# Two pairs of steps at a time in the attention loop of a fused attention, expert and gated kernel

## The chip, the cores and the metric

The kernel runs on one core of one Trainium2 chip. The metric is the device time of one execution in microseconds (us); lower is better. TensorE (PE) multiplies and transposes, VectorE (DVE) and ScalarE (ACT) do elementwise work, GpSimd (POOL) helps, and SyncE (SP) starts most transfers. Each engine takes its own instructions in the order in which they were written and waits for the others by semaphores.

## What is computed

The reference is attention with a window, then a layer in which each token goes to one of eight experts, then a gated layer. The part that the change touches is the attention and the choice of experts that hangs on it:

```python
scores = scale * np.matmul(q, k.transpose(0, 1, 3, 2))       # (4, 8, 768, 768), head_dim 64
keep = is_global | is_local                                  # 8 global keys, 96 local ones
scores = np.where(keep, scores + bias, -1000000000.0)        # bias: -slope of the head * distance
a = np.exp(scores - np.max(scores, axis=-1, keepdims=True))
a = a / (np.sum(a, axis=-1, keepdims=True) + 1e-09)
x = np.matmul(a, v)                                          # then 3072 tokens x 512
...
skip_score = x @ w_skip                                      # tokens with a positive one go on
e_idx = np.argmax(x @ w_gate, axis=1)
y = gate_w * (np.maximum(x @ w1[e], 0.0) @ w2[e])            # expert e of each token
...
return (gate * val @ w_out)                                  # gate, val: products of x with two weights
```

## The kernel before

**Steps and pairs.** The queries are cut into blocks of 128 rows. A step is one block of two heads. A batch has 24 steps (4 pairs of heads, 6 blocks each), and the four batches have 96. Two steps in a row are a pair, 48 pairs in all. Each block sees 256 keys (its own 128, 96 before it, 32 of the start); the first block of every pair of heads, step 0 of each six, sees only its own 128, so its products and elementwise work are half as wide. "Narrow step" means such a one below. Of three pairs in a row two hold a narrow step.

**What a pair goes through.** `scores(m)` (line 1785) makes the products of the two steps of pair m, eight matmuls that use 64 rows of the array each, two at a time (L1797). DVE's `lowest_of` (L911) adds the bias to a step's scores and takes the minimum of each row, into `score` and `lowest`. ACT's `exp_of` (L1510) makes `prob` and the sum of each row. `prob_transposes` (L1807) transposes a step's `prob` on PE, four transposes of 128x128. ACT's `pt_evac` (L1530) copies them to `probT`. `values(m)` (L1823) multiplies them with the values of the two heads, sixteen matmuls with 64 columns of the array each, two at a time, into `o_bank`. DVE's `take_heads_x` (L1117) copies that to `heads_x`. `turn(m)` (L1837) turns it to token rows and makes the expert scores in the same four matmuls, into `turned`. DVE's `take_rows` (L1011, L1131) reads `turned`, multiplies with the inverse sums (`guard_sums` L1107, `invert_sums` L1111) and stores to `head_logit` and `xs`.

**What sets the order.** It is written out by hand. PE's loop takes, for pair m: the scores of pair m+1, the transposes of pair m-1, the turn of pair m-2, the values of pair m-1. DVE takes two `lowest_of`, the sums of pair m-1, the rows of pair m-2, the copy of pair m-1. ACT takes two `pt_evac` of pair m-1 and two `exp_of` of pair m.

**What is shared.** `score`, `prob`, `probT` and `lowest` have a place for each of two steps; `lowest_of` of step n waits for the exp of step n-2. The four score places in PSUM (`sp_bank`) hold two pairs. `pt_bank` has two places: transposes of step n wait for `pt_evac` of step n-2 (`ptev_done`). `turned` is there once: `turn(m)` waits for the rows of pair m-1 (`oev_done`). The sums have two places, by pair: the exps of pair m wait for `guard_sums` of pair m-2 (`norm_chain`).

**Beside it**, per batch from the second on: `add_logits`, `choose` in three parts (seven small DVE instructions), `gate_exp` on ACT, `ranks` on PE (seven small matmuls, L1844 and L1846) with `take_ranks` and `gates` on DVE, all for the batch before. In the first batch `first_bias` and `window_bias` (L888) make the biases of the next pair of heads, after step 3 of each six.

## Time and profile before

| | |
|---|---|
| median of 3 runs | 966.11 us (966.04 to 967.0) |
| the profiled execution | 966.12 us, its span 964.5 us |
| around the span | 1.62 us |
| attention, from the first values to the last turn | 14.4 to 180.3 us of the span |
| PE, DVE, ACT busy over the whole span | 99%, 68%, 53% |
| PE, DVE, ACT busy from 20 to 170 us | 100%, 78%, 85% |
| granted PE clock | 1.00 throughout |

The expert layer and the gated layer follow the attention; they are not touched. PE's matmuls are pipelined and their ends are modelled, so a PE that is busy all the time by the table can still lose time between two kinds of matmul; that is read from the starts of single matmuls. In the rows below PE's time for a group of matmuls is therefore taken from start to start.

### The profile page before, as it was taken

The page shows a single profiled execution, that of the slowest core. Times are in us where ns is not written, and L with a number is a line of the kernel's source. Part 1 is how long each engine was busy: PE and PEld are TensorE (multiplying, and loading weights), DVE is VectorE, ACT ScalarE, POOL GpSimd, SP SyncE. Part 2 cuts the span into 40 slices and gives each one's busy share as a digit, 9 for nine tenths or more (in the row PEclk, how much of TensorE's full clock was granted, in tenths as well). Part 3 has the DMA queues.
Part 4 walks back from the last instruction along what each step waited for, and adds up shares of the span by engine and source line. Part 5 has one row for each costly group of instructions (what it writes and reads, how often), then busy time and mean ns, then how long its engine had stood idle before and what let it go on. Part 6 is the DMA issues. An engine that isn't in the chain of part 4 may idle for free.

```text
span 964.5 us, 16852 instructions
## 1 busy us (share of the span) xinstructions
PE 953.8 (99%) x5638; PEld 799.4 (83%) x5639; DVE 653.8 (68%) x1522; ACT 511.8 (53%) x1086; POOL 206.0 (21%) x229
## 2 busy tenths in 40 slices
PE   8999999999999999999999999999999999999998
PEld 6777777789999999788888888888888888888887
DVE  6887877675666266587677766676777846766653
ACT  5888888444444144364455554454555634545443
POOL 2405142722211111212323000323220013232100
PEclk9999999999999999999999999999999999999999
DMA  7677675689777265442211244512123432120242
GB/s 259 248 303 263 250 265 202 234 299 338 286 255 250 66 240 196 141 142 69 66 47 55 85 130 132 164 45 66 48 66 94 133 121 66 44 66 12 86 138 93
DMA packets 59660, 146.14 MB, mean 152 GB/s; under 512 B 6336, under 2 KB 12480, under 8 KB 59584
## 3 DMA queue, kind: packets, MB, share of 16 engines
q1 hardware_dynamic: 52624, 120.92, 37.5%
q0 software_dynamic: 6960, 24.27, 7.3%
q8 instruction: 40, 0.66, 0.3%
q14 instruction: 36, 0.29, 0.1%
HBM read 116.77 MB, written 28.40 MB: 151 GB/s over the span
## 4 chain that ended last, share of the span: by engine, by line
PE 96%; DVE 1%; DMA 1%; ACT 1%; issue 0%; SPq 0%; DVEq 0%; POOLq 0%; ACTq 0%
PE bank L2034 35%; PE bank L1781 14%; PE bank L1783 14%; PE bank L1782 14%; PE bank L1797 5%; PE bank L1807 5%; PE bank L1823 5%; PE bank L1837 2%; PE bank L2024 1%; PE bank L1962 1%; PE bank L1947 1%; DMA raw<-in_qk_dram 0%; DMA xq<-mixed 0%; PE bank L2087 0%; ACT prob L1510 0%
## 5 line engine op out<-in xcount | busy, mean ns | idle before, releaser
L2034 PE MATMUL bank<-xh,ws_h 128*128 128x512 f32 x490 | 190.6, 389 | 0.0
L2034 PE MATMUL bank<-xl,ws_h 128*128 128x512 f32 x490 | 190.6, 389 | 0.0
L2034 PE MATMUL bank<-xh,ws_l 128*128 128x512 f32 x490 | 190.6, 389 | 0.0
L845 POOL TENSOR_TENSOR p<-p,p 128x512 f32<-128x512 f32 x35 | 46.3, 1324 | 387.6 <-DVE p L1411 387.6
L1781 PE MATMUL bank<-woh,hh 128*128 128x512 f32 x288 | 112.9, 392 | 0.0
L1783 PE MATMUL bank<-woh,hl 128*128 128x512 f32 x288 | 112.2, 389 | 0.0
L1782 PE MATMUL bank<-wol,hh 128*128 128x512 f32 x288 | 112.1, 389 | 0.0
L2034 PEld LDWEIGHTS bank<-xh,ws_l 128*128 128x128 f32 x490 | 92.0, 188 | 19.1
L2034 PEld LDWEIGHTS bank<-xh,ws_h 128*128 128x128 f32 x490 | 92.0, 188 | 19.1
L2034 PEld LDWEIGHTS bank<-xl,ws_h 128*128 128x128 f32 x490 | 92.0, 188 | 19.1
L1510 ACT ACTIVATE prob<-score,lowest 128x256 f32<-128x256 f32 (+1 forms) x192 | 91.3, 482 | 6.2 <-DVE lowest L911 6.2
L1781 PE MATMUL bank<-sTh,w1h 128*128 128x256 f32 x288 | 80.7, 280 | 0.1
L1782 PE MATMUL bank<-sTl,w1h 128*128 128x256 f32 x288 | 80.4, 279 | 0.0
L1783 PE MATMUL bank<-sTh,w1l 128*128 128x256 f32 x288 | 80.4, 279 | 0.0
L1385 DVE TENSOR_TENSOR hl<-hid,hh 128x512 fp32r<-128x512 f32 x72 | 49.6, 689 | 44.1 <-ACT hh L1681 44.0
L1681 ACT ACTIVATE hh<-hid 128x512 fp32r<-128x512 f32 x72 | 45.2, 628 | 51.6 <-PE bank L1783 49.0
L1571 ACT ACTIVATE hTh<-bank 128x512 fp32r<-128x512 f32 x36 | 21.4, 595 | 90.4 <-PE bank L1783 89.9
L1530 ACT ACTIVATE probT<-bank 128x512 f32<-128x512 f32 (+1 forms) x96 | 51.0, 560 | 27.0 <-PE bank L1807 26.1
L911 DVE CUSTOM_DVE_ANT_0 score<-bank,bias_win 128x256 f32<-128x256 f32 x160 | 59.9, 421 | 7.9 <-issue 5.1
L1783 PEld LDWEIGHTS bank<-woh,hl 128*128 128x128 f32 x288 | 54.1, 188 | 11.4
L1781 PEld LDWEIGHTS bank<-woh,hh 128*128 128x128 f32 x288 | 54.1, 188 | 11.3 <-issue 0.5
L1782 PEld LDWEIGHTS bank<-wol,hh 128*128 128x128 f32 x288 | 54.1, 188 | 10.9
(266 smaller groups left out, 2005.5 us busy)
## 6 DMA issues: line engine op xcount, KB each, us to landing
wraw<-in_w_dram SPq DMA_DIRECT2D x64, 512.0 KB, 5.9
graw<-in_w_gated_dram SPq DMA_DIRECT2D x36, 512.0 KB, 3.6
woraw<-in_w_out_dram SPq DMA_DIRECT2D x72, 256.0 KB, 2.6
raw<-in_qk_dram SPq DMA_DIRECT2D x48, 336.0 KB, 6.2
vs<-in_own_prev_dram SPq DMA_DIRECT2D x16, 768.0 KB, 5.2
mixed<-xs SPq DMA_DIRECT2D x12, 512.0 KB, 3.2
xq<-mixed SPq DMA_DIRECT2D x12, 512.0 KB, 6.0
out_dram<-ostage SPq DMA_DIRECT2D x22, 256.0 KB, 2.0
```

What stands on the lines that cost most here:

```text
L845: pool.tensor_tensor(p7[:], p7[:], p1[:], ALU.add).then_inc(u3_done, 1)
L911: ins = dve.tensor_tensor_reduce(out=score[s % 2][:, t, lo:hi], in0=sp_bank[s % 4][t][:, lo:hi], in1=bias, scale=-HD ** -0.5, scalar=3e38, ...
L1385: dve.tensor_tensor(hl[u % 3][:], hid[:, c, h * HALF:(h + 1) * HALF], hh[u % 3][:].bitcast(f32), ALU.subtract).then_inc(hl_done, 1)
L1510: ins = act.activation(prob[s % 2][:, t, lo:hi], score[s % 2][:, t, lo:hi], ACT.Exp, bias=lowest[:, s % 2, t:t + 1], scale=-1.0, accum_out ...
L1530: act.activation(probT[n % 2][:, :, lo:2, :], pt_bank[n % 2][:].rearrange("p (t w c) -> p t w c", t=2, w=2)[:, :, lo:2, :], ACT.Copy).then ...
L1781: pe.matmul(dst, a_hi, b_hi, start=start, stop=False)
L1782: pe.matmul(dst, a_hi, b_lo, start=False, stop=False)
L1783: return pe.matmul(dst, a_lo, b_hi, start=False, stop=stop)
L1797: ins = pe.matmul(sp_bank[s % 4][t][:, lo:hi], both[half, i * P:(i + 1) * P], both[half, end - (hi - lo):end], start=True, stop=True)
L1807: ins = pe.transpose(pt_bank[n % 2][:, (2 * t + w) * P:(2 * t + w + 1) * P], prob[n % 2][:, t, w * P:(w + 1) * P], ident[:])
L1823: ins = pe.matmul(o_bank[t * HD:(t + 1) * HD, i * P:(i + 1) * P], vs[pr % 2][:, 1 - w, t, qi, :], probT[i][:, t, w, :], start=(w == 1 or q ...
L2034: ins = pe.matmul(bank, w[:, a + k], x[:, q, k], start=(first and k == 0 and i == 0), stop=(k == 1 and i == 2), skip_group_check=not first)
```

## The change

The loops of all three engines take two pairs (four steps) per turn, called a group below; a batch has 6 groups, and three groups in a row hold two narrow steps. PE takes the scores of two pairs (four steps), the transposes of the first two of the four steps before, the turn of a pair, the transposes of the third step, the turn of the next pair, the transposes of the fourth step, and the values of two pairs. DVE takes one copy of two pairs (128x512), four `lowest_of`, the sums of one pair, the rows of one pair, the sums of the next, the rows of the next. ACT takes four `pt_evac` and then four `exp_of`. `score`, `prob`, `probT` and `lowest` get four places instead of two, `heads_x` is one tensor of four blocks, and the values use the whole of `o_bank`. `pt_bank`, `turned` and the sums keep their places. The parts of `choose` stand behind the first three `lowest_of` of the batch's third group, the ranks in its fourth group. The semaphores' counts follow. After the last group the rest is written out.

```diff
@@ -118,7 +118,7 @@
-        lowest = small("lowest", [P, 2, 2], f32)
+        lowest = small("lowest", [P, 4, 2], f32)
...
+        more_probT = [till_ranks(f"probT{i}", [P, 2, 2, P], f32) for i in (2, 3)]
+        more_prob = [till_ranks("prob2", [P, 2, KW], f32, end=SMALL + 2 * UNIT + 4 * NQ * SLOT)]
...
-        heads_x = [att2(f"heads_x{i}", [P, 2, P], f32) for i in range(2)]
+        both_heads_x = att2("heads_x", [P, 2 * 2 * P], f32)
...
+        GROUPS = PAIRS // 2
+        CHOOSE, RANK, ROWS = 1, 3, 6
...
@@ -902,15 +912,15 @@
                 lo, hi = windows(qi)
                 n = STEPS * b + s
                 dve.wait_ge(s_done, n // 2 * 2 + 2)
-                if n >= 2:
-                    dve.wait_ge(exp_done, n - 1)
+                if n >= 4:
+                    dve.wait_ge(exp_done, n - 3)
                 alone(dve)
                 for t in range(2):
                     h = 2 * pr + t
                     bias = bias_0[:, h, :] if qi == 0 else bias_win[:, h, :]
-                    ins = dve.tensor_tensor_reduce(out=score[s % 2][:, t, lo:hi], in0=sp_bank[s % 4][t][:, lo:hi],
+                    ins = dve.tensor_tensor_reduce(out=score[s % 4][:, t, lo:hi], in0=sp_bank[s % 4][t][:, lo:hi],
                                                    in1=bias, scale=-HD ** -0.5, scalar=3e38, op0=ALU.add, op1=ALU.min,
-                                                   accum_out=lowest[:, s % 2, t:t + 1])
...
+            def take_heads_x(m, pairs):
+                dve.wait_ge(pv_done, m + pairs)
                 if m >= 2:
-                    dve.wait_ge(turned_done, m - 1)
-                dve.tensor_copy(heads_x[m % 2][:].rearrange("p s r -> p (s r)"), o_bank[:, 0:2 * P])\
-                   .then_inc(heads_x_in, 1)
+                    dve.wait_ge(turned_done, m + pairs - 2)
+                at = m % 2 * 2 * P
+                dve.tensor_copy(both_heads_x[:, at:at + 2 * P * pairs], o_bank[:, at:at + 2 * P * pairs])\
+                   .then_inc(heads_x_in, pairs)
...
-            def pair_after(m):
-
-                b, g = m // PAIRS, m % PAIRS
-                if 1 <= m <= NB * PAIRS:
-                    guard_sums(m - 1)
-                if 1 <= m <= NB * PAIRS:
-                    invert_sums(m - 1)
-                if m >= 2:
-                    take_rows(m - 2, (lambda: take_ranks(b)) if b and g == RANK else None)
-                if b and b < NB and g == CHOOSE:
-                    add_logits(b)
-                if b and b < NB and CHOOSE < g <= CHOOSE + 3:
-                    choose(b, g - CHOOSE - 1)
-                if b and g == RANK + 1:
-                    gates(b)
-                if 1 <= m <= NB * PAIRS:
-                    take_heads_x(m - 1)
+            def sums_inverted(m):
+                guard_sums(m)
+                invert_sums(m)
 
             def body(b):
+
                 if b == 1:
                     dve.wait_ge(const_ready, 1)
-                for s in range(STEPS):
-                    pr = s // NQ
-                    if b == 0 and pr and s % NQ < 2:
-                        dve.wait_ge(bias_done, 2 * pr + s % NQ + 1)
-                    if b or s > 1:
-                        lowest_of(b, s)
-                    if b == 0 and s % NQ == NQ - 3 and pr + 1 < NPAIR:
-                        first_bias(pr + 1)
-                        window_bias(pr + 1)
-                    if s % 2:
-                        pair_after(PAIRS * b + s // 2)
+                for g in range(GROUPS):
+                    m = PAIRS * b + 2 * g
+                    if m >= 4:
+                        take_heads_x(m - 4, 2)
+                    for s in range(4 * g, 4 * g + 4):
+                        pr = s // NQ
+                        if b == 0 and pr and s % NQ < 2:
+                            dve.wait_ge(bias_done, 2 * pr + s % NQ + 1)
+                        if b or s > 1:
+                            lowest_of(b, s)
+                        if b == 0 and s % NQ == NQ - 3 and pr + 1 < NPAIR:
+                            first_bias(pr + 1)
+                            window_bias(pr + 1)
+                        if b and g == CHOOSE + 1 and s % 4 < 3:
+                            choose(b, s % 4)
+                    if m >= 2:
+                        sums_inverted(m - 2)
+                    if m >= 4:
+                        take_rows(m - 4, (lambda: take_ranks(b)) if b and g == RANK else None)
+                    if m >= 2:
+                        sums_inverted(m - 1)
+                    if m >= 4:
+                        take_rows(m - 3)
+                    if b and g == CHOOSE:
+                        add_logits(b)
+                    if b and g == RANK:
+                        gates(b)
             batches(dve, body)
-            for m in range(NB * PAIRS, NB * PAIRS + 2):
-                pair_after(m)
+            end = NB * PAIRS
+            take_heads_x(end - 4, 2)
+            sums_inverted(end - 2)
+            take_rows(end - 4)
+            take_heads_x(end - 2, 1)
+            take_rows(end - 3)
+            sums_inverted(end - 1)
+            take_rows(end - 2)
+            take_heads_x(end - 1, 1)
+            take_rows(end - 1)
...
-                    ins = act.activation(prob[s % 2][:, t, lo:hi], score[s % 2][:, t, lo:hi], ACT.Exp,
-                                         bias=lowest[:, s % 2, t:t + 1], scale=-1.0,
+                    ins = act.activation(prob[s % 4][:, t, lo:hi], score[s % 4][:, t, lo:hi], ACT.Exp,
+                                         bias=lowest[:, s % 4, t:t + 1], scale=-1.0,
...
                 act.wait_ge(pt_done, n + 1)
-                if n >= 2:
-                    act.wait_ge(pv_done, n // 2)
+                if n >= 4:
+                    act.wait_ge(pv_done, n // 2 - 1)
                 lo = 1 if n % NQ == 0 else 0
-                act.activation(probT[n % 2][:, :, lo:2, :],
+                act.activation(probT[n % 4][:, :, lo:2, :],
...
             def body(b):
-                for g in range(PAIRS):
-                    m = PAIRS * b + g
-                    for i in range(2):
-                        if m >= 1:
-                            pt_evac(2 * m - 2 + i)
-                    for i in range(2):
-                        if m:
-                            exp_of(b, 2 * g + i)
-                    if b and g == CHOOSE + 2:
-                        gate_exp(b)
+                for g in range(GROUPS):
+                    n = STEPS * b + 4 * g
+                    for i in range(4):
+                        if n:
+                            pt_evac(n - 4 + i)
+                    for i in range(4):
+                        if n + i > 1:
+                            exp_of(b, 4 * g + i)
+                        if b and g == CHOOSE + 1 and i == 1:
+                            gate_exp(b)
             batches(act, body)
-            for i in range(2):
-                pt_evac(STEPS * NB - 2 + i)
+            for i in range(4):
+                pt_evac(STEPS * NB - 4 + i)
...
-                if m >= 1:
+                if m >= 2 and m % 2 == 0 or m == NB * PAIRS - 1:
                     pe.wait_ge(heads_x_in, m)
                 for i in range(2):
+                    at = (m % 2 * 2 + i) * P
                     qi = first + i
                     pe.wait_ge(ptev_done, 2 * m + i + 1)
                     for w in range(0 if qi else 1, 2):
                         for t in range(2):
-                            ins = pe.matmul(o_bank[t * HD:(t + 1) * HD, i * P:(i + 1) * P], vs[pr % 2][:, 1 - w, t, qi, :],
-                                            probT[i][:, t, w, :], start=(w == 1 or qi > 0) and (w == 0 or qi == 0),
+                            ins = pe.matmul(o_bank[t * HD:(t + 1) * HD, at:at + P], vs[pr % 2][:, 1 - w, t, qi, :],
+                                            probT[(2 * m + i) % 4][:, t, w, :], start=(w == 1 or qi > 0) and (w == 0 or qi == 0),
                                             stop=(w == 1))
                 ins.then_inc(pv_done, 1)
...
             def body(b):
-                for g in range(PAIRS):
-                    m = PAIRS * b + g
-                    if m + 1 < NB * PAIRS:
-                        scores(m + 1)
+                for g in range(GROUPS):
+                    m = PAIRS * b + 2 * g
+                    for i in range(2):
+                        if m + i:
+                            scores(m + i)
                     if m == 0:
                         keep_busy(4)
-                    if m >= 1:
-                        prob_transposes(2 * m - 2)
-                        prob_transposes(2 * m - 1)
-                    if m == 2:
+                    if m >= 2:
+                        prob_transposes(2 * m - 4)
+                        prob_transposes(2 * m - 3)
+                    if m == 4:
                         pe.wait_ge(router_loaded, 16)
                         pe.wait_ge(turner_ready, 1)
+                    if m >= 4:
+                        turn(m - 4, (lambda: ranks(b)) if b and g == RANK else None)
                     if m >= 2:
-                        turn(m - 2, (lambda: ranks(b)) if b and g == RANK else None)
-                    if m >= 1:
+                        prob_transposes(2 * m - 2)
+                    if m >= 4:
+                        turn(m - 3)
+                    if m >= 2:
+                        prob_transposes(2 * m - 1)
+                        values(m - 2)
                         values(m - 1)
                     if m == PAIRS:
                         pe.wait_ge(const_ready, 1)
             batches(pe, body)
             last = NB * PAIRS
+            prob_transposes(2 * last - 4)
+            prob_transposes(2 * last - 3)
+            turn(last - 4)
+            values(last - 2)
+            turn(last - 3)
             prob_transposes(2 * last - 2)
             prob_transposes(2 * last - 1)
             turn(last - 2)
```

How the rows stand on the engines, in the middle of the second batch. On PE, before, one pair and a half: L1797 scores, L1807 transposes, L1837 turn, L1823 values.

```order
L1807 MATMUL bank<-ident,prob_135 128x128 x4
L1807 MATMUL bank<-ident,prob_136 128x128 x4
L1837 MATMUL bank<-turner,heads_x_149 128x146 x2
L1823 MATMUL bank<-probT_137,vs_125 64x128 x4
L1823 MATMUL bank<-probT_138,vs_125 64x128 x4
L1797 MATMUL bank<-raw_132 128x256 x4
L1807 MATMUL bank<-ident,prob_135 128x128 x4
L1807 MATMUL bank<-ident,prob_136 128x128 x4
L1837 MATMUL bank<-turner,heads_x_148 128x146 x2
L1823 MATMUL bank<-probT_137,vs_125 64x128 x4
L1823 MATMUL bank<-probT_138,vs_125 64x128 x4
```

On PE, after, one group: L1819 scores (the second pair's), L1829 transposes, L1860 turn, L1846 values.

```order
L1819 MATMUL bank<-raw_135 128x256 x4
L1829 MATMUL bank<-ident,prob_138 128x128 x4
L1829 MATMUL bank<-ident,prob_139 128x128 x4
L1860 MATMUL bank<-turner,heads_x 128x146 x2
L1829 MATMUL bank<-ident,prob_124 128x128 x4
L1860 MATMUL bank<-turner,heads_x 128x146 x2
L1829 MATMUL bank<-ident,prob_162 128x128 x4
L1846 MATMUL bank<-probT_140,vs_128 64x128 x4
L1846 MATMUL bank<-probT_141,vs_128 64x128 x4
L1846 MATMUL bank<-probT_122,vs_128 64x128 x4
L1846 MATMUL bank<-probT_123,vs_128 64x128 x4
L1819 MATMUL bank<-raw_129 128x256 x4
```

Eight changes between kinds of matmul in two pairs become seven, but of those between different shapes of the array (64x128, 128x128, 128x64) six become three; the second turn stands behind the first with one step of transposes between them.

On DVE, before: the end of one `lowest_of`, the sums and rows of a pair, the copy, the next `lowest_of` (L911; each of its reads has a row of its own).

```order
L911 ISA score_134,lowest<-bank,bias_win 128x256 [waits s_done,exp_done]
L911 ISA lowest 128x1
L911 ISA score_134,lowest<-bank,bias_win 128x256
L911 ISA lowest 128x1
L1107 TENSOR_REDUCE rsum<-sums 128x4 [waits exp_done]
L1111 RECIPROCAL rsum<-rsum 128x4 [waits norm_chain]
L1011 TENSOR_TENSOR head_logit<-bank,rsum 128x2x2x9 [waits turned_done,norm_chain]
L1131 TENSOR_TENSOR xs_143<-bank,rsum 128x2x128
L1117 COPY heads_x_148<-bank 128x256 [waits turned_done,pv_done]
L911 ISA score_133,lowest<-bank,bias_147 128x128 [waits exp_done,const_ready,s_done]
```

On DVE, after: the fourth `lowest_of` of a group (L921), then sums, rows, sums, rows.

```order
L921 ISA score_161,lowest<-bank,bias_win 128x256 [waits s_done,exp_done]
L921 ISA lowest 128x1
L921 ISA score_161,lowest<-bank,bias_win 128x256
L921 ISA lowest 128x1
L1117 TENSOR_REDUCE rsum<-sums 128x4 [waits exp_done]
L1121 RECIPROCAL rsum<-rsum 128x4 [waits norm_chain]
L1021 TENSOR_TENSOR head_logit<-bank,rsum 128x2x2x9 [waits turned_done,norm_chain]
L1142 TENSOR_TENSOR xs_146<-bank,rsum 128x2x128
L1117 TENSOR_REDUCE rsum<-sums 128x4 [waits exp_done]
L1121 RECIPROCAL rsum<-rsum 128x4 [waits norm_chain]
L1021 TENSOR_TENSOR head_logit<-bank,rsum 128x2x2x9 [waits turned_done,norm_chain]
L1142 TENSOR_TENSOR xs_146<-bank,rsum 128x2x128
```

The rows of the first pair (L1021, L1142) now stand behind four `lowest_of` instead of two.

On ACT, before, two pairs: L1530 copies of transposes, L1510 exps.

```order
L1530 ACTIVATE probT_137<-bank 128x512
L1530 ACTIVATE probT_138<-bank 128x512
L1510 ACTIVATE prob_135,sums<-score_133,lowest 128x256 x2
L1510 ACTIVATE prob_136,sums<-score_134,lowest 128x256 x2
L1530 ACTIVATE probT_137<-bank 128x512
L1530 ACTIVATE probT_138<-bank 128x512
L1510 ACTIVATE prob_135,sums<-score_133,lowest 128x128 x2
L1510 ACTIVATE prob_136,sums<-score_134,lowest 128x256 x2
```

On ACT, after, one group: L1552 and L1532.

```order
L1552 ACTIVATE probT_140<-bank 128x512
L1552 ACTIVATE probT_141<-bank 128x512
L1552 ACTIVATE probT_122<-bank 128x512
L1552 ACTIVATE probT_123<-bank 128x512
L1532 ACTIVATE prob_138,sums<-score_136,lowest 128x128 x2
L1532 ACTIVATE prob_139,sums<-score_137,lowest 128x256 x2
L1532 ACTIVATE prob_124,sums<-score_156,lowest 128x256 x2
L1532 ACTIVATE prob_162,sums<-score_161,lowest 128x256 x2
```

All four exps of a group now stand behind the copy of the fourth step's transposes.

## Rows read from the trace of the kernel before

**Rows 1.** Busy time by stretch: stretch, then each engine's busy us (instructions), clock.

```profile
20.00:170.00 150.00, 150.00 (x1485) 118.74 (x1485) 117.66 (x600) 126.88 (x434) 47.15 (x59) 1.00 0.70 250
170.00:180.00 10.00, 8.35 (x83) 6.33 (x80) 6.39 (x31) 7.29 (x24) 9.82 (x7) 1.00 0.40 147
```

**Rows 2.** The chain of waits, three pairs: start us, us, what.

```profile
81.71 1.06 PE bank L1797 x8
...
85.32 1.06 PE bank L1797 x8
...
92.01 0.41 PE bank L1797
```

**Rows 3.** Instructions in order of time, PE: start us, us, engine, line, operation, count.

```profile
81.96 0.59 PE L1797 MATMUL bank<-raw 64*128 64x256 f32 x3
...
82.17 0.60 PE L1797 MATMUL bank<-raw 64*128 64x256 f32 x4
...
82.87 0.49 PE L1807 MATMUL bank<-ident,prob 128*128 128x128 f32 x3
...
83.63 0.41 PE L1837 MATMUL bank<-turner,heads_x 128*128 128x146 f32 x2
...
83.76 0.54 PE L1837 MATMUL bank<-turner,heads_x 128*128 128x146 f32 x3
84.22 0.55 PE L1823 MATMUL bank<-probT,vs 128*64 128x128 f32 x6
...
84.49 0.50 PE L1823 MATMUL bank<-probT,vs 128*64 128x128 f32 x6
```

**Rows 4.** Instructions in order of time, DVE, one narrow and one whole pair.

```profile
82.10 0.28 DVE L911 CUSTOM_DVE_ANT_0 score<-bank,bias 128x128 f32<-128x128 f32 x1
...
85.36 0.42 DVE L1117 COPY heads_x<-bank 128x256 f32<-128x256 f32 x1 [0.43 <-PE bank L1823]
85.71 0.41 DVE L911 CUSTOM_DVE_ANT_0 score<-bank,bias_win 128x256 f32<-128x256 f32 x1
...
87.08 0.16 DVE L1107 TENSOR_REDUCE rsum<-sums 128x4 f32<-128x8 f32 x1
87.27 0.18 DVE L1111 RECIPROCAL rsum<-rsum 128x4 f32<-128x4 f32 x1
87.80 0.20 DVE L1011 TENSOR_TENSOR head_logit<-bank,rsum 128x36 f32<-128x36 f32 x1 [0.35 <-PE bank L1837]
87.91 0.41 DVE L1131 TENSOR_TENSOR xs<-bank,rsum 128x256 f32<-128x256 f32 x1
```

**Rows 5.** Instructions in order of time, ACT: copies of transposes, exps.

```profile
83.39 1.08 ACT L1530 ACTIVATE probT<-bank 128x512 f32<-128x512 f32 x2 [0.62 <-PE bank L1807]
...
84.36 0.40 ACT L1510 ACTIVATE prob<-score,lowest 128x128 f32<-128x128 f32 x1
...
87.72 0.50 ACT L1510 ACTIVATE prob<-score,lowest 128x256 f32<-128x256 f32 x1
...
88.70 0.49 ACT L1510 ACTIVATE prob<-score,lowest 128x256 f32<-128x256 f32 x1
...
89.59 0.18 ACT L1510 ACTIVATION_READ_ACCUMULATOR prob<-score,lowest 128x1 f32 x1
```

**Rows 6.** Instructions in order of time, DVE: a minimum that waited for that exp.

```profile
89.95 0.42 DVE L911 CUSTOM_DVE_ANT_0 score<-bank,bias_win 128x256 f32<-128x256 f32 x1 [0.20 <-issue]
```

**Rows 7.** Instructions in order of time, DVE, first batch: biases, then the sums behind them.

```profile
12.83 0.49 DVE L888 SCALAR_TENSOR_TENSOR bias<-dist 128x128 f32<-128x128 f32 x2
...
13.91 0.15 DVE L1107 TENSOR_REDUCE rsum<-sums 128x4 f32<-128x8 f32 x1
```

**Rows 8.** Instructions in order of time, PE: start and end of the attention.

```profile
19.02 1.14 PE L1797 MATMUL bank<-raw 64*128 64x256 f32 x8
...
171.63 0.92 PE L1823 MATMUL bank<-probT,vs 128*64 128x128 f32 x12
...
179.86 0.77 PE L1837 MATMUL bank<-turner,heads_x 128*128 128x146 f32 x4 [0.53 <-DVE heads_x L1117]
```

19 lines of the change are left out of this document (12 added, 7 removed).

## The prediction

> **What bounds the kernel now.** I read four views in this order. First the busy time by stretch: from 20 to 170 us PE is busy for all 150 us, ACT for 126.88 and DVE for 117.66, at a clock of 1.00 [rows 1]. So PE sets the pace of the attention, and the two others have 15% and 22% to spare. Second the chain of waits: it runs through PE's scores, transposes, turn and values in turn, with 3.61 us from the scores of one pair to those of the next (81.71 to 85.32) and 10.30 for three pairs, two of them with a narrow step (81.71 to 92.01) [rows 2]. Two pairs take 6.87 us on average. Third the starts of single matmuls inside one whole pair [rows 3]; a row with xN starts N matmuls, so its first number is the start of the first. Fourth DVE's and ACT's instructions in order of time, for their lengths and for the delay from one engine to the next [rows 4 to 6].
>
> **What a pair costs on PE.** Slots, from start to start [rows 3]: scores 0.21 to 0.22 per two matmuls (81.96 to 82.17), 0.216 taken; transposes 0.109 (82.87 to 83.63 is seven); turn 0.125 (83.63, 83.76); values 0.109 per two matmuls, the same 128 columns. A whole pair is 4 x 0.216 + 8 x 0.109 + 4 x 0.125 + 8 x 0.109 = 3.11 us. The other 0.50 of the 3.61 is lost where the shape of the array changes. From turn to values: the last turn starts at 84.01, the third double matmul of the values at 84.49, and 0.48 less 0.125 and two slots is 0.14. From scores to transposes: 82.39 to 82.87, less 0.216 and two slots with rounding, 0.15. From values to scores the rest, 0.20.
>
> **What the change takes away.** Two pairs have each of these three seams once instead of twice: 0.50 us per group. With 24 groups that is 12.0 us. This holds only if nothing new makes PE wait, and the next part says that something does. The four places for scores, probabilities and transposes remove waits that are short today, the larger buffers cost nothing, and the single copy of 512 columns (two of 0.42 today [rows 4]; between 0.42 and 0.84, I take 0.7) ends before the new scores can be read.
>
> **What the change adds: a wait at the second turn.** `turned` exists once. The second turn of a group waits until DVE has taken the rows of the first, and on DVE these rows stand behind the copy and all four minima of the group. Lengths: a minimum 0.69 per step (85.71 to 87.08 is two); sums 0.37 (87.08 to the end of the reciprocal); rows 0.53 (87.80 to 88.32) [rows 4]. Delay from PE's last start to DVE 0.32 (the last values start at 85.04, the copy at 85.36). I take 0.06 from DVE back to PE; no row isolates it, 0 to 0.1 bounds it.
>
> *The loop through DVE*, from one second turn to the next, all steps whole: turn 0.50, transposes 0.44, seam 0.14, values 16 x 0.109 = 1.74, seam 0.20, four slots of scores up to the last start 0.65, delay 0.32, four minima 2.74, sums 0.37, rows 0.53, back 0.06: 7.69 us. *The loop through ACT*: turn 0.50, last transpose starting 0.33 later, delay to ACT 0.32, copy 0.49 (two take 1.08 less the overlap, 83.39 to 84.36), four exps 3 x 0.98 + 1.07 = 4.01 (87.72, 88.70, end 89.77), to the minimum that waits for the last exp 0.17 (89.95), that minimum 0.69, sums 0.37, rows 0.53, back 0.06: 7.47 us [rows 5, 6]. PE itself would need 6.22 + 0.50 = 6.72. So either loop is longer than PE's work, and today's 7.22 for two whole pairs too.
>
> A narrow step takes 0.22 from its values, 0.21 from its scores where it stands in the group's first pair, 0.27 from its minimum (0.28 against 0.42 [rows 4], twice) and 0.2 from its exp (0.40 against 0.50 [rows 5], twice). Three groups in a row have a narrow step at their start, in their third step, and nowhere. Over three intervals DVE's loop then gives 7.42 (a narrow minimum), 7.47 (narrow values), 6.99 (all three), and ACT's 7.27, 7.27, 7.47. The longer one decides: 7.42 + 7.47 + 7.47 = 22.36 us against 20.60 today. The attention has 22 such intervals between its first and last full group: 164.0 against 151.1, **+12.9 us**.
>
> **What loses its cover.** Today DVE's extra work hides beside PE; in the new order it stands between minima or behind them, in the loop that decides. Biases of the first batch, two sets inside the intervals, 1.08 each (12.83 to 13.91 [rows 7]): +2.2. `choose`, seven small instructions of some 0.18 (the reciprocal [rows 4]), three times: +3.8. Ranks: their seven matmuls (7 x 0.109, about 0.8) lie on PE's path today and beside DVE's loop then; instead `take_ranks` and `gate_exp` enter it, three small instructions, some 0.6: -0.2, three times, -0.6. `add_logits` and `gates` stand behind the second rows, where DVE waits for the values anyway: nothing.
>
> **Start and end.** Today the first two pairs' values are done by 19.0 us [rows 8]. In the new order the exps of steps 2 and 3 no longer stand behind two copies, but the second pair of scores does stand ahead of the first transposes; between -1 and +1, I take -0.5. At the end, today, 7.4 us lie between the end of the last values but two (some 172.5) and the last turn (179.86) [rows 8]. In the new order the last four exps end 2.8 us after the values of the last full group, a copy of transposes starts at 2.7, values at 3.4 to 4.4, two transposes and a turn to 6.4, the last copy of transposes ends at 6.7, values at 7.6, DVE's copy at 8.3: +1.0. The work behind the attention waits for this last turn and moves with it.
>
> Sum: 12.9 + 2.2 + 3.8 - 0.6 - 0.5 + 1.0 = +18.8 us. The profiled execution took 966.12 us (its span 964.5 and 1.62 around it, which I leave as it is), and the median is 966.11: 984.9.
>
> **Rivals.** *PE's seams decide, 954.1.* If the second turn didn't have to wait, the gain of 12.0 would stand. For it: the seams are in the rows, and DVE and ACT are idle 22% and 15% of the stretch. Against it: the idle time is there on average, but the loops above have their delays in series. It decides once both loops are under 6.7 us, one whole microsecond shorter than worked out. The Trainium skill, page TensorEngine Tiling, section Key Properties, says that changing the tiling mode drains TensorE; the seams of this trace, 0.14 to 0.20, agree with it, and by that rule alone the change is a gain.
>
> *Both loops are shorter, 966 to 976.* If DVE's loop is 0.5 shorter than I have it (shorter handoffs), ACT's still holds: 22 intervals at 7.34 are 161.4, +10.3, and with the other terms 982. Only if ACT's is 0.3 shorter as well do they fall to 7.04 and the time to about 976. No row supports it.
>
> *The clock falls, about 1010.* PE would stand still for about 1 us in each group. Should the granted clock go to 1.2 GHz for a sixth of the stage, four groups' PE work of 6.7 us doubles: +27. Against it: from 170 to 180 us PE was busy 8.35 of 10 us and the clock stayed at 1.00 [rows 1]. On that the Trainium skill, page TensorE: Matmul & The Clock Gate, section HAM oscillation, has a rule that idle gaps between matmul bursts lower the clock; here no row shows it.
>
> *The change does nothing, 966.* Only if loop and seams cancel: intervals of 6.9 and all extra work hidden. I see no reason.
>
> **Chances.** Forecast 0.80; seams decide 0.08; in between, faster or slower, 0.07; the clock or a longer loop 0.05. The unknown terms (handoffs 0.05 x 22, start 1, choose 1, copy 0) make the likeliest case 979 to 992; I give 976 to 994. Faster by over 0.2% 0.09, within 0.2% 0.03 (0.2%, some 2 us, is about what a measurement can tell), slower 0.88.
>
> **What would show it.** Right: the transposes and values of a group are separated from the turn by a wait of PE for DVE's `xs` at the second turn, some 1 us in nearly every group; second turns 7.4 to 7.5 us apart, some 8.7 where `choose` stands; PE busy 85 to 90% in the stage; seams once per two pairs; the expert and gated stages as long as before. Wrong: no idle PE at the second turn, or the stage shorter than 166 us.

## The result, and the profile after

The changed kernel takes 1004.15 us (median of six runs, 1000.58 to 1006.45), the kernel before 966.43 in the same comparison (966.04 to 967.83). The ratio is 1.0385, with a 95% interval of 1.036 to 1.041: slower by 37.7 us, where 18.8 were predicted, and above the range's 994. The profiled execution has a span of 999.7 us, 35.2 more than before. All of it lies in the attention: the last turn starts at 214.98 us instead of 179.86 [rows 8], 35.1 later, and what follows is as long as it was.

The busy time by stretch is the view that answers [rows 1]. The columns are the stretch, the busy us of PE, PE's weight loads, DVE, ACT and POOL, then the clock, the share of the transfer engines and GB/s:

```profile
20.00:170.00 150.00, 123.14 (x1220) 104.05 (x1218) 94.71 (x482) 103.27 (x355) 39.85 (x45) 0.97 0.57 207
170.00:180.00 10.00, 7.21 (x62) 5.99 (x58) 6.62 (x33) 5.33 (x20) 0.44 (x2) 0.87 0.74 264
126.30:129.60 3.30, 3.30 (x30) 2.97 (x28) 0.69 (x1) 3.30 (x15) 0.00 (x0) 0.50 0.40 86
```

PE is busy for 82% of the stage instead of all of it. The clock is no longer 1.00: from 126.3 to 129.6 us, for instance, it is 0.50, which is the lower of its two levels, 1.2 GHz. There are six such stretches in the attention, about 3.4 us each, starting at 13.5, 34.0, 126.2, 143.2, 177.4 and 204.7 us. The waits from 20 to 200 us (engine, line, whom it waited for: total us, times, longest):

```profile
PE bank L1860 <- DVE xs L1142: 29.6, 20, 2.8
```

L1860 is the turn and L1142 the rows. So the predicted wait is there, at the predicted place, and in nearly every group, but it is 1.5 us long on average and not 1. The chain of waits, which answers [rows 2], goes through one group like this (start us, us, what; only its larger pieces):

```profile
43.10 0.73 PE bank L1860 x4
43.84 0.44 PE bank L1829 x4
44.27 1.68 PE bank L1846 x28
45.95 1.09 PE bank L1819 x8
...
47.24 0.25 DVE score L921
...
50.48 0.34 DVE xs L1142
50.82 0.14 issue
50.96 0.74 PE bank L1860 x4
```

That is the loop through DVE as the prediction drew it: second turn, last transposes, values, the scores of one pair, then the four minima, sums and rows, and the next second turn. The same group as instructions in order of time, PE first (it answers [rows 3]), then DVE [rows 4] and ACT [rows 5]; in square brackets is the idle time ahead and what ended it:

```profile
43.10 0.73 PE L1860 MATMUL bank<-turner,heads_x 128*128 128x146 f32 x4 [1.27 <-DVE xs L1142]
43.67 0.60 PE L1829 MATMUL bank<-ident,prob 128*128 128x128 f32 x4
44.20 1.75 PE L1846 MATMUL bank<-probT,vs 128*64 128x128 f32 x28
45.88 2.00 PE L1819 MATMUL bank<-raw 64*128 64x256 f32 x16
...
50.96 0.74 PE L1860 MATMUL bank<-turner,heads_x 128*128 128x146 f32 x4 [1.30 <-DVE xs L1142]
```

```profile
46.06 0.69 DVE L1128 COPY heads_x<-bank 128x512 f32<-128x512 f32 x1 [1.58 <-issue]
47.24 0.42 DVE L921 CUSTOM_DVE_ANT_0 score<-bank,bias_win 128x256 f32<-128x256 f32 x1 [0.50 <-PE bank L1819]
...
50.01 0.16 DVE L1117 TENSOR_REDUCE rsum<-sums 128x4 f32<-128x8 f32 x1
...
50.40 0.41 DVE L1142 TENSOR_TENSOR xs<-bank,rsum 128x256 f32<-128x256 f32 x1
```

```profile
44.31 0.60 ACT L1552 ACTIVATE probT<-bank 128x512 f32<-128x512 f32 x1 [1.85 <-PE bank L1829]
44.80 0.50 ACT L1532 ACTIVATE prob<-score,lowest 128x256 f32<-128x256 f32 x1
```

DVE's rows are as long as before. The single copy of 512 columns took 0.69 us, as taken, and DVE idles 0.50 us behind it, so the copy isn't on the path. The time between two second turns, called the interval below, is 7.86 us (43.10 to 50.96).

By the starts of all second turns, intervals free of falls of the clock and of extra work are 7.55 to 7.86 us, those with the three parts of choose 9.2 to 9.3, those with the biases 8.6, those with the ranks 8.2. Some are 8.3 to 9.6 for two further reasons, which the experiments separate.

The biases, on DVE, as in [rows 7]; they stand between the last minimum and the sums, 1.07 us from 31.66 to 32.73:

```profile
31.66 0.49 DVE L898 SCALAR_TENSOR_TENSOR bias<-dist 128x128 f32<-128x128 f32 x2
...
32.73 0.15 DVE L1117 TENSOR_REDUCE rsum<-sums 128x4 f32<-128x8 f32 x1
```

Start and end of the attention on PE, as in [rows 8]:

```profile
18.90 2.00 PE L1819 MATMUL bank<-raw 64*128 64x256 f32 x16
...
214.98 0.77 PE L1860 MATMUL bank<-turner,heads_x 128*128 128x146 f32 x4 [0.53 <-DVE heads_x L1128]
```

### The profile page after: what moved, and what is told of

Same layout as the page of the kernel before. It is cut to its first block, busy times and chain, and to the rows that moved or that the text cites. A ratio compares the mean times of both kernels' runs of the same rounds, so it can differ in the third digit from the quotient of the medians.

```text
span 999.7 us, 16791 instructions
## 1 busy us (share of the span) xinstructions
PE 954.2 (95%) x5638; PEld 809.2 (81%) x5639; DVE 650.4 (65%) x1499; ACT 510.4 (51%) x1086; POOL 205.6 (21%) x229
## 4 chain that ended last, share of the span: by engine, by line
PE 85%; DVE 7%; ACT 4%; issue 3%; DMA 1%; DVEq 0%; ACTq 0%; POOLq 0%; SPq 0%
PE bank L2069 33%; PE bank L1803 13%; PE bank L1805 13%; PE bank L1804 13%; DVE score L921 4%; ACT prob L1532 3%; PE bank L1846 3%; PE bank L1860 2%; PE bank L1819 2%; PE bank L1829 2%; DVE xs L1142 1%; PE bank L1997 1%; PE bank L2059 1%; PE bank L1982 1%; DMA xq<-mixed 0%
## 5 line engine op out<-in xcount | busy, mean ns | idle before, releaser
L2069 PEld LDWEIGHTS bank<-xl,ws_h 128*128 128x128 f32 x490 | 92.0, 188 | 18.8
L1532 ACT ACTIVATE prob<-score,lowest 128x256 f32<-128x256 f32 (+1 forms) x192 | 91.1, 478 | 6.9 <-DVE lowest L921 6.9
L1552 ACT ACTIVATE probT<-bank 128x512 f32<-128x512 f32 (+1 forms) x96 | 51.0, 555 | 62.5 <-PE bank L1829 57.8
L1860 PE MATMUL bank<-turner,heads_x 128*128 128x146 f32 x192 | 35.4, 309 | 33.3 <-DVE xs L1142 31.6
L921 DVE CUSTOM_DVE_ANT_0 score<-bank,bias_win 128x256 f32<-128x256 f32 x160 | 58.9, 420 | 9.5 <-PE bank L1819 8.5
```

The source lines that it names most:

```text
L921: ins = dve.tensor_tensor_reduce(out=score[s % 4][:, t, lo:hi], in0=sp_bank[s % 4][t][:, lo:hi], in1=bias, scale=-HD ** -0.5, scalar=3e38, ...
L1532: ins = act.activation(prob[s % 4][:, t, lo:hi], score[s % 4][:, t, lo:hi], ACT.Exp, bias=lowest[:, s % 4, t:t + 1], scale=-1.0, accum_out ...
L1552: act.activation(probT[n % 4][:, :, lo:2, :], pt_bank[n % 2][:].rearrange("p (t w c) -> p t w c", t=2, w=2)[:, :, lo:2, :], ACT.Copy).then ...
L1860: ins = pe.matmul(turned[:, i], heads_x[m % 2][:, i], turner[:, pr], start=True, stop=True)
L2069: ins = pe.matmul(bank, w[:, a + k], x[:, q, k], start=(first and k == 0 and i == 0), stop=(k == 1 and i == 2), skip_group_check=not first)
```

## The experiments

Each comparison has runs of the kernel before on the same chip beside it; ratios are to those. There were thirteen runs: twelve other kernels, and the changed kernel once more.

### Only the places (e3)

The kernel before with four places for scores, probabilities and their transposes, and nothing else of the change.

> The kernel before in its own order, with only the four places for score, prob, probT and lowest of the changed one and the waits loosened to match. Theory A: TensorE sets the pace and the waits for places are short, so 965 to 967 us. If the new places themselves cost something (another layout in memory): above 968.

965.9 us (964.3 to 966.95), ratio 0.9993 (0.9983 to 1.0003). The larger buffers cost nothing, as the prediction had it. The whole loss is in the order.

### The first rows earlier (e1)

```diff
+                        if s % 4 == 1 and m >= 4:
+                            take_rows(m - 4, (lambda: take_ranks(b)) if b and g == RANK else None)
                     if m >= 2:
                         sums_inverted(m - 2)
-                    if m >= 4:
-                        take_rows(m - 4, (lambda: take_ranks(b)) if b and g == RANK else None)
```

> The changed kernel with one edit on VectorE: the rows of a group's first pair are taken behind the group's second minimum instead of behind the fourth and the sums. Theory A (the loop through VectorE and the wait at the second turn make the kernel slow, and the idle TensorE there also lets its clock fall): the waits at the second turn shrink from some 1.5 us to under 0.6, no stretch of the attention runs at half clock, intervals between second turns fall to 6.9 to 7.1 us where nothing extra stands, and the time to 969 to 975 us. Theory B (taking four steps at a time is itself too long for the two places of pt_bank and for ScalarE, whatever VectorE's order): intervals stay at 7.5 or more and the time above 985.

970.8 us (969.45 to 973.63), ratio 1.0053 (1.0034 to 1.0072). One call moved by two minima takes 33 of the 37.7 us back (32 by the ratios). The wait at the second turn, from 20 to 170 us:

```profile
PE bank L1860 <- DVE xs L1142: 7.7, 16, 0.7
```

The second turns are 6.87 to 7.17 us apart (8.0 to 8.3 in the groups with ranks), and there is no stretch at half clock in the attention. So the wait for the rows behind four minima is the cause of nearly all of it, the falls and the late signals with it; how it comes to cost twice what was predicted is the question of the next runs.

### Filling the wait (e2, e5)

Matmuls of no use stand ahead of each second turn, so that PE is busy while it waits; nothing else changes. First 12 (26 in the groups with choose), then, since the first was too long, 4 (and 10):

```diff
+            def warm(n):
+                for _ in range(n):
+                    pe.matmul(o_bank[:, 0:P], ident[:], ident[:], start=True, stop=True)
...
                     if m >= 4:
+                        if not (b and g == RANK):
+                            warm(10 if b and g == CHOOSE + 1 else 4)
                         turn(m - 3)
```

> The changed kernel with extra matmuls (128x128 by 128 columns, result unused) on TensorE ahead of each second turn, 12 in a normal group, 26 in the groups with choose, none in the groups with ranks: they fill the time in which TensorE stands still, and change no dependency. Theory A with the clock: the clock stays at 1.00 from the first filled group on, and the five stretches of 3.4 us at half clock, which lengthened intervals by 0.7 to 1.5 us, are gone: 995 to 999 us. If the clock costs nothing because TensorE waits anyway: 1002 to 1006. If the fill itself delays the turn: above 1006.

1019.8 us (1019.05 to 1022.78), ratio 1.0549: slower, the third case of the expectation, in which the fill itself delays the turn. So this run can't decide between the two theories. The trace shows why (PE, in order of time):

```profile
59.53 2.84 PE L1803 MATMUL bank<-ident 128*128 128x128 f32 x24
62.21 0.66 PE L1864 MATMUL bank<-turner,heads_x 128*128 128x146 f32 x4
```

Each float32 matmul of the text is two on the engine, so 12 became 24 of 0.112 us, 2.7 us where 1.3 to 1.5 were free. The fill set the pace, with intervals of 9.0 to 9.4 us, and 12.1 in the groups with choose. The clock stayed at 1.00 after the first 17 us, all the same.

> The changed kernel, with matmuls of no use put ahead of the second turn of each group: 4 of them (8 passes in the trace, each 0.112 us as in the run with the long fill, 0.90 us together), 10 in the three groups with choose (2.24 us), none in the groups with the ranks. In the run with the long fill the number of passes was twice what I had reckoned (24 for 12 matmuls), 2.7 us where PE waits 0.8 to 1.6, so that the fill itself set the pace. The short one fits into the wait. Theory that the long waits bring the clock down: no stretch at half clock after the first turns, each of the six stretches of the changed kernel gave away about 1.4 us, so 994 to 997. Rival, the falls have nothing to do with the waits: stretches at half clock remain and the time is 1001 to 1006. If the fill still delays the turns: intervals over 7.9 and a time above 1004.

997.0 us (996.77 to 999.68), ratio 1.0303 (1.0284 to 1.0322), within the expectation. From 20 to 200 us the changed kernel and this one show, in this order:

```profile
20.00:200.00 180.00, 148.08 (x1460) 125.09 (x1457) 112.08 (x570) 123.78 (x428) 49.15 (x61) 0.96 0.58 209
```

```profile
20.00:200.00 180.00, 165.38 (x1669) 143.80 (x1670) 115.80 (x591) 125.22 (x431) 54.74 (x64) 1.00 0.59 213
```

The clock is 1.00 in place of 0.96. The fill does no useful work, and where no fall was, the intervals are what they were (7.85 and 7.80 us in both traces) or 0.16 longer (7.71 for 7.55). So the 7 to 8 us by which it is faster are what the falls of the clock cost. The intervals say the same: four that hold a fall in the first trace and none here are 0.5 to 1.6 us longer there, and the first second turn comes 1.0 us later. It doesn't say what PE must do to keep the clock, only that with most of each wait filled (up to 1.5 us of idle time was left) it stays.

### Choose behind the rows (e4)

`choose` moved from between the minima to behind the second rows, with `gate_exp` two exps later.

> The changed kernel with the three parts of choose behind the second rows of their group instead of between its minima, and the gate's exp behind the group's last exp. Theory A: the three intervals of 9.2 to 9.3 us fall to 7.8 to 8.2, 1.2 us each, and with the longest idle times of TensorE (2.9 us) some of the half-clock stretches behind them go: 996 to 1001 us. If choose is hidden in both places: 1003 to 1006.

991.1 us (990.09 to 993.06), ratio 1.0257 (1.0235 to 1.0279), better than either number. The three groups with choose went from 9.2 to 7.9 us each, 4 us as expected. The longest waits of all, 2.7 to 2.8 us, stood in these groups, and some falls were expected to go with them; more went than was reckoned. There are two stretches at half clock instead of six, both in the first 40 us. What the expectation didn't have is that the late signals, below, did not occur in this trace either: the two ordinary intervals of 8.49 us are 7.85 here, those of 8.93 and 8.26 are 7.81. GpSimd's transfers are as bunched as in the changed kernel (six from 86.0 to 93.1 us, the last four 1.26 us after each other).

### The same kernel once more (e8)

> The changed kernel unaltered, a second profiled execution. If the stretches at half clock and the late handoffs (at 94.8 to 95.9, 138 to 140, 191 and 198 to 200 us in the first trace) belong to the program, they stand at the same places. If they depend on the execution, some stand elsewhere, and the last turn is not at 215.0 but some us off, as the runs' spread from 1000.6 to 1006.5 suggests; the intervals without either are 7.55 to 7.85 in both.

1002.6 us. The last turn starts a microsecond earlier than in the first trace. Stretches at half clock start at 32.8, 124.9, 142.0 and 176.1 us, each within 1.3 us of one of the first trace; those at 13.5 and 204.7 are missing, and one stands behind the attention, at 442.4. The long intervals stand in the same groups. So which wait brings a fall is mostly the program's, and a few are settled by the execution. The six runs spread over 5.9 us, those of the kernel before over 1.8, and the granted clock over the whole run goes with their times: 0.991 at 1000.58 us, 0.985 at 1006.31 and 1006.45.

### The late signals and the bunched transfers (e6, e7, e9 to e11)

In the first trace four intervals are long without any wait that the order explains. One of them, on PE, DVE and POOL:

```profile
196.31 1.75 PE L1846 MATMUL bank<-probT,vs 128*64 128x128 f32 x28
197.99 2.00 PE L1819 MATMUL bank<-raw 64*128 64x256 f32 x16
```

```profile
199.39 0.69 DVE L1128 COPY heads_x<-bank 128x512 f32<-128x512 f32 x1 [2.81 <-issue]
```

```profile
193.51 0.96 POOL L766 DMA_INDIRECT row_table<-xs,row_i  x1 [1.63 <-DVE lowest L921]
194.77 0.96 POOL L766 DMA_INDIRECT row_table<-xs,row_i  x1 [0.30 <-issue]
196.03 0.96 POOL L766 DMA_INDIRECT row_table<-xs,row_i  x1 [0.30 <-issue]
197.30 0.96 POOL L766 DMA_INDIRECT row_table<-xs,row_i  x1 [0.30 <-issue]
```

The copy waits only for the values, whose last matmul starts 0.2 us ahead of the scores at 197.99. Elsewhere it starts 0.18 us behind the first scores (45.88, 46.06), here 1.40. PE had started the work, and its signal came late. GpSimd was writing the rows of the batch before at that time, four indirect transfers 1.26 us after each other. They hang on DVE's minima (`low_done`): in the kernel before the three pairs start 3.4 us apart; in the new order minima come in bursts of four and the transfers with them.

I first saw how much this can cost in two variants that should have been better than the one with the rows earlier. One moves the extra work of `choose` and the ranks as well, the other also puts the second turn behind all transposes:

```diff
                         turn(m - 4)
                     if m >= 2:
                         prob_transposes(2 * m - 2)
+                    if m >= 2:
+                        prob_transposes(2 * m - 1)
                     if m >= 4:
                         turn(m - 3, (lambda: ranks(b)) if b and g == RANK else None)
                     if m >= 2:
-                        prob_transposes(2 * m - 1)
                         values(m - 2)
```

> The changed kernel with the first rows behind the group's second minimum (as in e1), and the extra work moved as well: choose behind the second rows, gate_exp behind the fourth exp, the ranks ahead of the second turn and take_ranks ahead of the second rows. In e1 the groups with the ranks took 8.0 to 8.3 us where the others took 6.87 to 7.17, and there were three. Theory (extra work in the loop from turn to rows to turn counts, beside it it doesn't): three times 1.0 us less, 967 to 968.5. Rival, the ranks' seven matmuls cost the same wherever they stand on PE: 970 to 971.

985.0 us (981.59 to 987.82), ratio 1.0163: 14 us slower than what it was made from (e1), 11 by the ratios.

> As e6, and the second turn moved behind the transposes of the fourth step, so that eight transposes instead of four lie between the two turns (four steps' transposes, then seam, then values). In e1 PE waits 0.6 to 0.9 us at the second turn for rows that come 1.45 us after the start of the first turn, with 0.5 of turn and 0.44 of transposes in between. Theory: another 0.44 of work in between takes 0.44 off each of 22 intervals, 9.7 us less than e6, as far as PE's own 6.3 us allow: 957 to 960, and with it the seams' gain shows at last. Rival: the transposes of the fourth step wait for ScalarE's second copy instead (pt_bank has two places), the wait only moves, and the time stays at e6's 967 to 968.

978.6 us (977.24 to 981.87), ratio 1.0099. The ordinary intervals do fall, to 6.37 to 7.06 us in this one, but one group of each batch takes 11 to 13.6 us in both. From 81 to 84 us, first with the extra work moved (e6), then with the rows alone moved (e1):

```profile
81.00:84.00 3.00, 0.28 (x4) 0.19 (x4) 0.53 (x2) 0.84 (x2) 2.49 (x3) 0.97 1.02 388
```

```profile
81.00:84.00 3.00, 3.00 (x36) 2.36 (x33) 1.49 (x7) 3.00 (x14) 2.54 (x3) 1.00 1.01 389
```

PE stands still in e6, in the middle of its values, for nothing that a wait names:

```profile
83.81 1.12 PE L1847 MATMUL bank<-probT,vs 128*64 128x128 f32 x8 [2.72 <-issue]
```

Its signals reach the others 2 to 5 us late, those of the other engines on time. The transfer engines are full in both traces, and the six indirect transfers start at the same times (75.9 to 82.5 us); so they are a condition, and not the whole cause. The test was to pull the pairs of transfers apart, in e7 (e9), in the changed kernel (e10), and there with the short fill as well (e11):

```diff
-                    if b and ROWS <= g < ROWS + NQ // 2:
+                    if b and g in (ROWS, ROWS + 2, ROWS + 4):
                         pool.wait_ge(low_done, 2 * (PAIRS * b + g) + 4)
-                        scatter(b, range(2 * (g - ROWS), 2 * (g - ROWS) + 2))
+                        scatter(b, range(g - ROWS, g - ROWS + 2))
```

> As e7, with the three pairs of indirect transfers of each batch (the rows of the batch before, written out by GpSimd's queue) a whole group of four minima apart, instead of two pairs behind each other. In the kernel before the pairs start 3.4 us apart, in e7 six transfers start 1.3 us after each other, and it is there, in one group per batch, that the intervals are 12.8, 11.0 and 13.0 us instead of 6.4 to 7.0: PE stands still for nothing that the profile shows and its signals come 2.6 to 5.1 us late. Theory (the bunched transfers are the cause, together with the loads that fill the transfer engines): those three intervals fall to about 7, no stretch at half clock is left, 978.6 less some 16 to 17 gives 961 to 963, under the kernel before. Rival (the loads or GpSimd's splitting of weights are the cause, wherever the transfers stand): the long intervals stay, or move to another group, 974 to 980.

969.9 us (967.15 to 970.74), ratio 1.0018 (1.0008 to 1.0028). The three intervals fell from 12.8, 11.0 and 13.0 us to 6.8, 7.1 and 6.9, as expected. The gain by the medians is 8.7 us and not 16. The 16 had been read from e7's trace, and that is its slowest run (981.87, against a median of 978.57); it and e9's trace, which is its fastest run, differ by 14.7. A stretch at half clock also stands at 174 us now, near the end of the attention, behind waits of 0.33 and 0.95 us.

> The changed kernel with the same single edit as in e9. Theory: the late signals of TensorE at 94.8 to 95.2, 138 to 139, 191 and 198 to 199 us go, the intervals of 8.49, 8.93, 8.26 and 8.49 us fall to 7.6 to 8.0, 3 us less than the changed kernel and perhaps one stretch at half clock fewer, 999 to 1001. Rival: no effect, 1001 to 1005.

1000.0 us (996.88 to 1002.64), ratio 1.0331: 4 us less by the medians, 5 by the ratios. The time is as expected, the intervals only in part. Two of the four, of 8.49 us, fell to 7.85, and so did a third of 9.5 us that had held a fall of the clock too. Those of 8.9 and 8.3 us stayed. One group that took 8.2 us in both traces of the changed kernel took 11.0, with 6.8 us at half clock. Since two of four long intervals stayed with the transfers apart, and e4 had the transfers in bursts and none of the four, bunched transfers are neither needed for a late signal nor enough for one.

> The changed kernel with both edits that changed nothing of its order of turns and rows: the short fill of e5 and the transfers apart of e10. What is left is the wait itself. By itself the fill gave 997 and the spacing 1000. If the falls of the clock and the late signals are two causes that add, this gives 992 to 994.5, with no stretch at half clock, and intervals of 7.6 to 7.9 but for the biases (8.6), choose (9.2) and the ranks (8.1). If they overlap (the late signals cost only by the falls they bring): 996 to 998.

994.1 us (993.83 to 995.01), ratio 1.0281 (1.0265 to 1.0296). Both edits count beside each other; the spacing is worth 3 us on top of the fill (2 by the ratios). This is nearly the changed kernel with the waits of its order alone: 27.1 us over the kernel before, which had 967.03 here. Its runs lie within 1.2 us. The two intervals of 8.9 and 8.3 us are still there, 1.6 us in all over their like.

### Does the seams' gain exist? (e12, e13)

With the turn last and the transfers apart the order has no wait of note left, and still was no faster than before. Two more steps. In e12 the sums of the first pair and the first rows stand behind the second minimum, the second rows behind the third:

> As e9, with DVE's sums of the first pair behind the group's second minimum, ahead of the first rows, and the second rows behind the third minimum. In e9 ScalarE's exps wait 0.4 to 0.7 us for the sums in most groups (the places of the sums come free late), the transposes then wait for the exps, and the intervals stay at 6.37 to 7.06 where PE's own work is 6.2 to 6.7. Theory: the exps start earlier, some 0.1 to 0.2 us less in each of 22 intervals, 966 to 968. Rival, PE's own work is already the bound there: 969 to 970.5, as e9.

968.2 us (965.28 to 969.7), ratio 1.0006 (0.9996 to 1.0015). The attention ends 2.9 us earlier than in the kernel before, and what follows is 4.9 us longer. One step of choose, while GpSimd splits x (DVE, then POOL):

```profile
180.77 1.85 DVE L1054 SCALAR_TENSOR_TENSOR pick<-ldiff,weight_id 128x48 f32<-128x48 f32 x1
```

```profile
180.76 1.80 POOL L791 TENSOR_TENSOR lastl<-xs,lasth 128x768 fp32r<-128x768 f32 x1
```

In e13 the second and third pair of transfers stand two minima sooner.

> As e12, with the second and the third pair of each batch's indirect transfers two minima sooner (behind the 18th and 22nd minimum of the batch instead of the 20th and 24th; still 3.8 and 7 us apart). In e12 the attention's last turn starts at 177.0 us, 2.9 earlier than in the kernel before (179.9), yet the span is 966.5 against 964.5. What follows the last turn is 4.9 us longer: GpSimd waits for these transfers of the fourth batch until 174.1 before it splits the last x, its TENSOR_TENSOR (180.8 to 182.6) then lies beside DVE's choose, of which one step takes 1.85 us instead of 0.21, TensorE waits 2.5 us for it, and a stretch at half clock follows at 185.8. Theory: with the transfers two minima sooner GpSimd starts some 1.5 to 2 us sooner, the long step shrinks to 0.3, the stretch at half clock goes: 963 to 965.5, under the kernel before. Rival (the tail is longer for another reason): 967 to 969, as e12.

964.75 us (963.11 to 967.16), ratio 0.9973 (0.9962 to 0.9985), within the expectation and the one version that beats the kernel before, which had 967.78 beside it. The same pair of rows now:

```profile
179.73 0.21 DVE L1055 SCALAR_TENSOR_TENSOR pick<-ldiff,weight_id 128x48 f32<-128x48 f32 x1
```

```profile
177.50 1.82 POOL L792 TENSOR_TENSOR lastl<-xs,lasth 128x768 fp32r<-128x768 f32 x1
```

The last turn starts at 176.4 us, 3.4 earlier than before. Ordinary intervals are 6.37 to 6.72 us where two pairs of the kernel before take 6.69 to 7.0; three in a row are 19.5 to 19.8 us against 20.6, so 0.3 to 0.4 us less per group. In three groups each change of shape stands three times instead of six, and costs what it did (from the last start of one kind to the first of the next 0.31, 0.22 and 0.20 us in both traces). So the gain by the seams is there, but it isn't the whole 0.50; where the rest goes was not followed. Groups with choose, ranks and late signals are 6.9 to 8.2 us long. No run gave the kernel before the transfers of e13.

## Why the prediction was wrong

**The bound, and what the change takes away: right.** PE set the pace, the larger buffers cost nothing, and the seams are worth something only where no wait takes their place. The two rivals in which the wait is absent or short fall.

**The wait at the second turn: right in place and mechanism, short by 0.3 to 0.4 us in size.** In the group shown, values with one narrow step, the prediction had 7.47 and the trace has 7.86. Term by term, the trace first: from the turn to the values 1.10 (43.10 to 44.20) against 1.08; values to the first scores 1.68 against 1.73; from the first scores to the first minimum 1.36 (45.88 to 47.24) against 0.97; the minima 2.77 against 2.74; sums and rows 0.80 against 0.90; back to PE 0.15 (50.81 to 50.96) against 0.06. The step that failed is "Delay from PE's last start to DVE 0.32". It was read at the copy, which waits for matmuls of the values, and used for the minimum, which waits for scores. In the trace the signal of the last of the four scores comes at 47.04, and the minimum starts 0.20 us behind it, where the copy of [rows 4] started 0.02 behind the signal of the values (85.34, 85.36). Also, scores of 256 columns are 0.38 us long by the trace, and values 0.27. The other 0.1 is in the seam, part of which lies behind the first scores. The way back had been bounded at 0 to 0.1 without a row, and is 0.15. Over 22 intervals that is some 6 us. The run with fill and spacing (e11) bears it out. Its last turn starts at 206.55 us, 26.7 later than in the kernel before; less the 1.6 of late signals that is 25.1, where the prediction had 18.8, so 6.3 more.

The loop through ACT doesn't set the time of the group shown. In every third interval, where all three parts have a narrow step, it has a share, as the prediction said: the minima wait for exps there (DVE):

```profile
104.07 0.29 DVE L921 CUSTOM_DVE_ANT_0 score<-bank,bias 128x128 f32<-128x128 f32 x1 [0.29 <-ACT prob L1532]
```

These intervals are 7.55 to 7.70 us, against 7.47.

**Biases, choose, ranks: right.** 1.07 per set of biases against 1.08, choose 1.4 to 1.5 a group against 1.3, ranks 0.5 to 0.6 against 0.6.

**Start and end: small, and the end right.** In the first trace the start is only 0.1 us earlier (18.90 against 19.02), but a stretch at half clock lies ahead of it and another one over the last full group's values. Without them (e11, PE) the start is 1.3 earlier, where 0.5 was taken, and from the end of the last full group's values to the last turn it is 8.4 us against 7.3, 1.0 longer as predicted:

```profile
17.75 2.00 PE L1823 MATMUL bank<-raw 64*128 64x256 f32 x16
...
196.43 1.75 PE L1850 MATMUL bank<-probT,vs 128*64 128x128 f32 x28
...
206.55 0.77 PE L1864 MATMUL bank<-turner,heads_x 128*128 128x146 f32 x4 [0.53 <-DVE heads_x L1128]
```

**The clock: the rival that was rated at 0.05 came true, in a smaller size.** The prediction argued from [rows 1] that PE at 8.35 of 10 us had kept the clock at 1.00. That row is true and says little: there the idle time lay in short pieces, and here one wait of 0.6 to 2.8 us stands in each group. The stretches at half clock begin at the end of long waits or up to 1.5 us behind them:

```profile
124.70 0.74 PE L1860 MATMUL bank<-turner,heads_x 128*128 128x146 f32 x4 [2.66 <-DVE xs L1142]
125.27 0.60 PE L1829 MATMUL bank<-ident,prob 128*128 128x128 f32 x4
125.80 2.96 PE L1846 MATMUL bank<-probT,vs 128*64 128x128 f32 x28
```

These 28 matmuls took 1.75 us at 44.20. The rule of the Trainium skill, page TensorE: Matmul & The Clock Gate, section HAM oscillation, that idle gaps between bursts lower the clock, agrees with this trace in its direction; the gaps of that section's own kernel are longer than any wait here, and waits of 1.6 to 2.8 us brought falls here. Not each long wait did it: the one that ends at 75.7, in a group with choose as well, was followed by a fall in neither trace of the changed kernel, though in e10 a fall of 6.8 us began within it (at 73.9). The falls cost 7 to 8 us (e5).

**What no step had: the late signals,** 4 to 5 us (e10), or 2 to 3 with the falls already filled (e11 against e5: 997.0 to 994.1). The prediction moved no transfer in its thinking, since GpSimd's text is unchanged. But GpSimd's transfers hang on `low_done`, and the change alters when that counts.

**The sum.** 18.8 predicted; 6 for the mis-sized handoffs; 7 to 8 for the clock; 2 to 5 for the late signals: 34 to 38, against 37.7. The handoffs alone give 991, inside the range; it is the clock, rated at 0.05, and the transfers, which had no term, that take the time out of it. The range had added up the handoffs and the start as unknowns (0.05 x 22), but left the clock outside as unlikely, and had nothing for the transfers.

**Open.** Why PE's signals come late, and PE stops at times, is not settled. Spacing the indirect transfers removed the worst cases (e7 to e9), yet e1 had the same transfers at the same times and ran undisturbed, e4 had them in bursts and ran undisturbed as well, and two long intervals of the changed kernel stayed with them apart (e10). Why the minimum starts 0.20 us behind its signal and the copy 0.02 is not tested either. No run left the transfers or the loads out, so their share isn't known apart.

## What to carry to other kernels

Before an order is changed so that a buffer with one place comes free only behind a longer piece of another engine's work, add up the whole loop in series, with each handoff read at the very pair of instructions that it joins: a handoff is counted from the producer's end, and that depends on its length. Move the small step that frees the buffer ahead of the long work (here one call, 33 us). Also look for engines that the change doesn't name but whose waits count its steps, here GpSimd's transfers, which went from even spacing to bursts.

## What the runs showed of the hardware

- In the changed kernel TensorE's clock fell to half for 3.4 us (6.8 once in e10) at or behind some waits of 1.6 to 2.8 us, and not behind others as long, although PE was busy for 82% of the stage. The length of one wait doesn't decide it: with waits of up to 0.7 us in the loop and one of 1.4 at 178 us (e1) it didn't fall, and in e9 it fell at 174.1 us behind waits of 0.3 and 0.95. With short matmuls of no use in the waits (8 of 0.11 us where 1.3 to 1.5 us were free) it stayed at 1.00.
- With indirect transfers in a burst and the transfer engines full, PE stood still for 2.7 us in the middle of its matmuls with no wait named (e6), and its signals came 2 to 5 us late; those of DVE, ACT and GpSimd did not. The same transfers at the same times in e1 brought none of this.
- A DVE operation on 128x48 elements took 1.85 us beside a TENSOR_TENSOR of GpSimd that ran for 1.80 us at the same time (e12), and 0.21 with GpSimd's out of its way (e13). In e12 it ended at 182.62, GpSimd's at 182.56. That agrees with the Trainium skill, page SBUF — State Buffer, section on the two separate sides: a DVE operation with two SBUF inputs and a GpSimd one that reads SBUF share a port pair, and whichever starts first has it for its whole instruction. The same section says that TensorE never waits on anyone in SBUF and that no transfer slows an engine; whether the standstill above goes against that is open, since its cause is.
- A float32 matmul of the program text that isn't a transpose is two on the engine, 0.112 us each at 128 columns (e2: 24 for the 12 in the text).
